# Which queue issues tile 1's keys and queries, and one zero product ahead of the first scores

## The reference

```python
scores = scale * np.matmul(q, k.transpose(0, 1, 3, 2))
keep = is_global | is_local          # 8 global keys, 96 local ones
scores = np.where(keep, scores + bias, -1e9)
a = exp(scores - max); a = a / (sum(a) + 1e-9); x = np.matmul(a, v)
h = x @ w_in; solu = h * softmax(h)
x = layer_norm(solu) * g_ln @ w_out
h = x @ w_in2; return (h * sigmoid(h)) @ w_out2
```

## Time and profile before

| | us |
|---|---|
| median of 3 runs | 492.46 (492.1 to 492.82) |
| the profiled execution | 491.45 |
| its span, first to last instruction | 489.4 |
| TensorE busy | 481.3 |
| VectorE, ScalarE, GpSimd busy | 303.5, 267.2, 228.9 |

### The profile page before, as it was taken

The page is one execution under the profiler, slowest core; times in us unless marked ns, Lnnn a source line. Parts: engine busy times, 40 slices in busy tenths (PEclk is TensorE's granted clock), DMA queues, the critical chain, the costliest instruction groups (busy, mean ns, idle before and its releaser), DMA issues.

```text
span 489.4 us, 8015 instructions
## 1 busy us (share of the span) xinstructions
PE 481.3 (98%) x2757; PEld 413.4 (84%) x2757; DVE 303.5 (62%) x729; ACT 267.2 (55%) x591; POOL 228.9 (47%) x304
## 2 busy tenths in 40 slices
PE   8989999999999999999999999999999999999997
PEld 6667888888888878888899988988899998988995
DVE  6877755675666777666575658565565546545542
ACT  5888556475566565745854454454454454344422
POOL 6626308779779779431624431444125431444100
PEclk9999999999999999999999999999999999999999
DMA  7994012642641641402222202221016202220003
GB/s 208 253 266 122 18 33 71 159 114 49 160 129 41 154 124 38 126 0 88 86 87 87 87 4 83 86 87 49 39 65 238 86 4 83 87 86 1 1 1 129
DMA packets 20522, 44.38 MB, mean 91 GB/s; under 512 B 2624, under 2 KB 8704, under 8 KB 20480
## 3 DMA queue, kind: packets, MB, share of 16 engines
q1 hardware_dynamic: 20160, 43.47, 30.7%
q10 hardware_dynamic: 320, 0.37, 0.3%
HBM read 40.69 MB, written 3.15 MB: 90 GB/s over the span
## 4 chain that ended last, share of the span: by engine, by line
PE 68%; POOL 18%; issue 4%; DVE 4%; SPq 3%; DMA 2%; ACT 1%; POOLq 0%
PE hidden_ps L1192 24%; PE score_ps L1215 9%; POOL k_split L703 7%; PE x_ps L1027 6%; POOL probs L730 5%; PE x_t_ps L1215 5%; PE x_ps L1215 5%; PE probs_t_ps L1215 5%; PE turn_ps L1215 5%; PE hidden_ps L978 3%; POOL k_split L701 3%; DVE solu L1763 2%; POOL q_lo L717 2%; DMA staged_q_raw<-q_t 2%; PE x_t_ps L965 2%
## 5 line engine op out<-in xcount | busy, mean ns | idle before, releaser
L873 POOL TENSOR_TENSOR wo_lo<-w_raw,wo_hi 128x512 fp32r<-128x512 f32 x32 | 41.4, 1312 | 145.6 <-ACT wo_hi L1461 145.6
L1473 ACT ACTIVATE act_hi<-mix_c 128x384 fp32r<-128x384 f32 x64 | 33.7, 526 | 96.5 <-DVE mix_c L1852 96.2
L730 POOL TENSOR_SCALAR probs<-probs,exp_inv 128x232 f32<-128x232 f32 x88 | 40.2, 474 | 43.6 <-DVE exp_inv L1623 41.6
L1295 ACT ACTIVATE probs<-logits,low_logit 128x232 f32<-128x232 f32 x96 | 45.5, 477 | 3.2 <-DVE low_logit L1610 2.9
L1852 DVE TENSOR_TENSOR mix_u<-hidden_ps,mix_p 128x384 f32<-128x384 f32 x16 | 8.9, 558 | 57.0 <-PE hidden_ps L1192 57.0
L1027 PE MATMUL x_ps<-w_out_hi,u_hi 128*128 128x512 f32 x96 | 40.5, 422 | 0.0
L1857 DVE TENSOR_TENSOR act_lo<-mix_c,act_hi 128x384 fp32r<-128x384 f32 x64 | 36.1, 567 | 6.3 <-ACT mix_c L1474 5.5
L1027 PE MATMUL x_ps<-w_out_hi,u_lo 128*128 128x512 f32 x96 | 37.9, 395 | 0.0
L1027 PE MATMUL x_ps<-w_out_lo,u_hi 128*128 128x512 f32 x96 | 37.6, 391 | 0.0
L978 PE MATMUL hidden_ps<-w_in_hi,x_hi 128*128 128x512 f32 x80 | 33.0, 412 | 0.0
L1474 ACT ACTIVATE mix_c<-mix_c 128x384 f32<-128x384 f32 x64 | 32.5, 508 | 0.0
(11 more groups left out here) (215 smaller groups left out, 1456.8 us busy)
## 6 DMA issues: line engine op xcount, KB each, us to landing
w_raw<-w SPq DMA_DIRECT2D x16, 1024.0 KB, 5.0
v_sb<-v_win SPq DMA_DIRECT2D x22, 224.0 KB
late_k_raw<-k_t SPq DMA_DIRECT2D x16, 232.0 KB, 4.4
k_raw<-k_t SPq DMA_DIRECT2D x14, 232.0 KB, 3.8
out<-out_sb SPq DMA_DIRECT2D x12, 256.0 KB, 2.1
w_in_raw<-w_in SPq DMA_DIRECT2D x4, 512.0 KB, 8.3
w_out_raw<-w_out SPq DMA_DIRECT2D x4, 512.0 KB, 12.4
late_q_raw<-q_t SPq DMA_DIRECT2D x16, 128.0 KB, 4.1
```

The costliest lines, as they stand in the source:

```text
L730: last = nc.gpsimd.tensor_scalar(probs[p][:, e, :], probs[p][:, e, :], exp_inv[:, p, e:e + 1], 0.0, ALU.mult, ALU.add)
L873: nc.gpsimd.tensor_tensor(wo_lo[j % 2][:, c, :], w2_raw[j % 2][:, c, BANK:2 * BANK], wo_hi[j % 2][:, c, :].bitcast(F32), ALU.subtract).the ...
L1295: last = nc.scalar.activation(probs[p][:, e, :], logits[b][:, e, :], ACT.Exp, scale=-1.0, bias=low_logit[:, b, e:e + 1], accum_out=exp_sum ...
L1473: nc.scalar.activation(act_hi[c][:, :], mix_c[c][:, :], ACT.Silu)
```

## The change

The function `load_early` moves out of SP's block so that any engine can run it, and takes the engine as an argument. The call for tile 1 is taken out of SP's list and put into ScalarE's, behind `load_first(act, 0)` and ahead of `first_table(0)`; the calls for tiles 2, 3 and 4 stay with SP. The first `keep_warm` has six products of zeros instead of seven.

```diff
--- before.py
+++ after.py
@@ -551,21 +551,20 @@
             eng.dma_start(staged_k_raw[rows, keys], k_v[0, unit][:, keys]).then_inc(loaded, 16)
             eng.dma_start(staged_q_raw[rows, queries], q_v[0, unit][:, queries]).then_inc(loaded, 16)
 
+    def load_early(eng, t):
+
+        if t in (2, 3):
+            eng.wait_ge(scores_done, PAIRS * (t - 1))
+        keys, queries = raw_of(t, 0)
+        for unit in range(2):
+            eng.dma_start(keys[unit * DH:unit * DH + DH, :], k_v[t, unit]).then_inc(early_loaded[t], 16)
+        for unit in range(2):
+            eng.dma_start(queries[unit * DH:unit * DH + DH, :], q_v[t, unit]).then_inc(early_loaded[t], 16)
+
     with nc.Block() as block:
 
         @block.sync
         def _(sp):
-            def load_early(t):
-
-
-                if t in (2, 3):
-                    sp.wait_ge(scores_done, PAIRS * (t - 1))
-                keys, queries = raw_of(t, 0)
-                for unit in range(2):
-                    sp.dma_start(keys[unit * DH:unit * DH + DH, :], k_v[t, unit]).then_inc(early_loaded[t], 16)
-                for unit in range(2):
-                    sp.dma_start(queries[unit * DH:unit * DH + DH, :], q_v[t, unit]).then_inc(early_loaded[t], 16)
-
             def load_keys_queries(t, s):
 
                 if not there(t):
@@ -615,7 +614,6 @@
 
             sp.dma_start(spans_i[:, :], spans).then_inc(spans_loaded, 16)
             load_first(sp, 1)
-            load_early(1)
             load_values(0, 0)
             load_values(0, 1)
             load_weight(0)
@@ -631,15 +629,15 @@
                 sp.dma_start(wide_q[:, :], wide_q_v[0, 0, 0]).then_inc(wide_stored, 16)
                 wide_heads(sp, wide_head)
             load_wide_x(0)
-            load_early(2)
+            load_early(sp, 2)
             load_weight(4)
             load_weight(5)
-            load_early(3)
+            load_early(sp, 3)
             load_values(2, 0)
             load_values(2, 1)
             load_weight(6)
             load_weight(7)
-            load_early(4)
+            load_early(sp, 4)
             load_keys_queries(WHOLE, 0)
             load_wide_x(1)
             load_wide_x(2)
@@ -1150,7 +1148,7 @@
             for _ in range(5):
                 nc.tensor.matmul(turn_ps[:, 0:P], x_hi[:, 0:P], x_hi[:, 0:P], start=True, stop=True)
             pe.wait_ge(zeros_made, 1)
-            keep_warm(7)
+            keep_warm(6)
             early_scores(0, 0)
             early_scores(0, 1)
             pe.wait_ge(identity_made, 1)
@@ -1484,6 +1482,7 @@
                                      bias=wide_stat[:, 0:1], accum_out=wide_stat[:, 1:2]).then_inc(wide_exp_done, 1)
 
             load_first(act, 0)
+            load_early(act, 1)
             first_table(0)
             first_table(1)
             exps(0, 0)
```

## The result

The changed kernel takes 494.58 us (median of 6 runs, 493.7 to 495.52) against 492.01 of the kernel before (6 runs, 491.48 to 492.82). The ratio is 1.0047, with a 95% interval of 1.0031 to 1.0062: slower, and outside the range given. The profiled execution took 494.52, its span is 492.5, which is 3.1 more than before. The medians lie only 2.6 apart: the profiled execution of the kernel before (491.45) was quicker than its median, so differences between the two sets of rows can come out some 0.5 us too large.

The account below looks back on a forecast made before the run. Loads bound the stage: tile 2's scores start at the later of A (25.46 - 0.30 = 25.16) and B (24.85), so 0.30 us earlier, taking the 492.46 median to 492.2 us. The 8-in-10 range was 491.4 to 493.2.

Parts of the forecast that it names:

- A: Time when tile 2 has landed and its scores can start: 25.46 before, forecast 25.16.
- B: Time when TensorE has finished the work ahead of tile 2's scores: 24.55 before, forecast 24.85.
- 0.91 of cover: TensorE's wait for tile 2's load, 24.55 to 25.46, claimed to hide delays in earlier work.
- no drain behind the table load: ScalarE's next activation follows the table load at once; the skill page's drain would make the kernel 0.8 us slower.
- the late first mask: VectorE's first mask at about 7.72 instead of 7.42, waiting for ScalarE's late bias tables: +0.30 us on following work.
- the product's place: One zero product fewer on TensorE: tile 0's first scores 0.46 us earlier, at 4.88, a gain not used later.
- the landing of tile 1: Tile 1's keys and queries, through ScalarE's queue, land at 9.5 instead of 10.4; harmless up to 10.7.
- Rival 3: ScalarE's queue gets only half the engines; tile 1 landing from 11.3 on costs time, at 12.2 493.35 us; chance 0.12.
- the favourable bound: Best case for tile 1's loads: data alone takes 3.0 us, so 8.0 plus a tail of 0.3 to 1.1.
- the second half of tile 0: Load for tile 0's later scores, taken as landed at 6.15, before the first half's passes end.
- rival 4: TensorE idle from 9.0 to 12.2 gets the lower clock again: up to 3 us, 495.5; chance 0.05.
- two stretches in which the engines were not full: DMA holes at 5.50 to 6.00 and 10.25 to 11.25, worth 0.20 and 0.23 us; filling them gains 0.30.

Follow-up runs that it names:

- SP held back: Changed kernel, but SP waits for tile 0's landing before issuing values and weights: 491.95 us, ratio 0.9992 to the kernel before; repeated, 491.74, ratio 0.9996.
- one-queue kernel: Kernel before with six zero products, SP issuing tile 1's loads behind tile 0's values instead of ahead: 493.4 us against 492.66, ratio 1.0018.
- split kernel: Changed kernel, but ScalarE issues unit 0 of tile 1 and SP unit 1 ahead of the values: 492.16 us against 492.66, ratio 0.9984.
- second experiment: Changed kernel with seven zero products put back, so only the loads move: 494.78 us, ratio 1.0045 to the kernel before.
- first experiment: Kernel before with six zero products instead of seven, tile 1's loads still on SP: 491.89 us against 492.16, ratio 0.9993.
- third experiment: Changed kernel with six more zero products between tile 0's score halves and twelve more before tile 1's scores: 493.63 us, ratio 1.0025 to the kernel before.
- the one that waits behind the values: Changed kernel, but SP issues tile 0's values, then waits for tile 0's landing before the first weight load: 493.93 us, ratio 1.0031 to the kernel before.

## Why the prediction was wrong

**Right.** That the stage is max(A, B) with 0.91 of cover in the profiled execution, and that TensorE runs almost through behind it. (Its waits of over 0.2 us do not all end by 32.50: the fifth, of 0.23 for GpSimd, ends at 172.03. It changes nothing.) The issue times (table load at 5.95 for 5.91; four issues of 0.62 with 0.04 between them are 2.60, as measured, and not 2.56), no drain behind the table load, the first scores at 4.92 for 4.88, the late first mask (7.88 for 7.72), and that the product's place brings nothing. With SP held back, ScalarE's late start costs what was worked out: TensorE was ready for tile 2 at 25.14 - 0.20 = 24.94 and at 26.09 - 1.10 = 24.99, for a B of 24.85.

**The step that failed** is the landing of tile 1. I took 9.5 "as the values ahead of it in SP's queue are only 0.48 MB", with 12.2 as the worst. It was 13.1. The 9.5 does not even follow from that premise: 0.74 and 0.48 MB at the 247 GB/s of the sum are 4.9 us, so 9.9 and, with the tail of 0.3 to 1.1, 10.2 to 11.0. The one-queue kernel, with just these values ahead, had tile 1 at 12.4. The larger error is in what shares the engines: not the loads ahead in the other queue, but all that this queue holds until the last byte lands, the weights behind the values included. The fair comparison was 0.75 MB of ScalarE's and 1.06 MB of SP's, over the 8 us that they took together. That the weights share in the delay follows from this count (1.06 MB is more than the 0.48 MB of values); no run held back the weights alone until tile 1 had landed. Rival 3 had the mechanism and its threshold (11.3), with a chance of 0.12 and a landing still 0.9 too early. By its own rule 13.1 gives B = 24.85 + 2.4 = 27.25, and +1.8; what the landing adds in the profiled execution, 2.67 less the 0.91 of cover, is about the same 1.8. Its chance was too low because I read the 28% for ScalarE's queue from 4.50 to 5.25 as a queue that had little left, and let the favourable bound stand nearer.

**A second miss** lies under it: the second half of tile 0 was taken as landed at 6.15, as before. It landed at 8.2. I had asked what shares the engines with the moved loads, and not what the moved loads share them with. Its wait of 1.46 us has no price of its own in these rows, as tile 1 came later still, but it is nearly all of the 1.69 us of idle time ahead of the clock's fall.

**The clock** was rival 4, tied to an idle stretch from 9.0 to 12.2 and given 0.05. It fell at 9.9, ahead of the wait for tile 1: behind the wait of 1.46 for tile 0's second half, the scores of that half and 0.23 more. It stayed low to 16.7, with the 1.93 of waiting for tile 1 inside. The split kernel had the same kind of wait for tile 0 (1.53), none for tile 1, and its clock was back by 13.0. Of the 4.0 us by which TensorE is behind at 16.98, 2.67 are there when tile 1's scores start, and 1.34 come in the stretch at the lower clock (scores 1.92 for 1.05, and the turn and zero products behind them). Less the cover of 0.91 that is 3.1, close to the growth of the span. The fall doesn't happen in every execution to the same degree: mean clocks were 0.992 to 0.997 in the changed kernel's runs, which lie 1.8 apart, and 0.989 to 0.999 in those of the second experiment, 3.8 apart. The two rivals were also not apart: late landings, tile 0's first of all, bring the idle time, and so their chances should have been one chance with both prices.

**Tile 2's landing (A)** was forecast 0.30 earlier, from two stretches in which the engines were not full. It came later instead:

```profile
L562 SPq DMA_DIRECT2D staged_q_raw<-q_t x1: 597/597/597, 13.0 to 13.0; - x1
...
DMA to landing us min/median/max: 13.7/13.7/13.7
```

Tile 2 landed at 13.0 + 13.7 = 26.7 in the profiled execution, 1.3 later than before. There it no longer mattered, as TensorE came at 28.47. But it means that even with B as forecast this execution would have started tile 2's scores 1.2 us late and not 0.30 early. Part of that may be the difference between executions, as the other kernels have 25.14 to 26.09 for a start that waits on this load. The first stretch did not fill: the DMA share from 2.00 to 6.50 is 0.71, where it was 0.85. Why more issued loads left the engines emptier is open; from 4.75 to 6.25 the one-queue kernel has 0.70 against 0.88 of the kernel before, so it is not the second queue as such.

## What to carry to other kernels

A second queue is no second set of engines. Before a load is moved to it, add up all that the first queue will hold from the issue of the moved load to its landing, and give each queue a share of the engines: a load on which an engine waits belongs where nothing unneeded is served beside it. Here a wait of the other queue on the urgent data, one line, brought back the whole loss. And where an engine's clock depends on its work, a wait that becomes longer can cost twice: once as the wait, and once in the slower work behind it. Count the waits of the loads that share engines with the moved ones too.

## What the runs showed of the hardware

The lower clock came although TensorE had been busy for half of the stretch before it (1.71 of 3.40 us). In the first experiment it was busy for 1.89 of the same 3.40 us (6.50 to 9.90), and the clock stayed at 1.00. The times spread more where the clock fell: 492.9 to 496.66 in the second experiment, with mean clocks of 0.989 to 0.999, against 493.1 to 494.2 where zero products filled the waits. That the clock is the whole reason is not shown: the second experiment's run at 0.999 took 495.54, and the kernel before lay between 490.74 and 494.36 in one session, with clocks of 0.995 to 1.0. The Trainium skill (TensorE: Matmul & The Clock Gate, section "Part 1: The HAM clock gate (the "warmup" mystery)") says that the throttled state is the default, which activity releases, and that the moment differs from run to run for the same kernel. The traces agree. Two kernels with the same work on TensorE up to the end of these passes, the third experiment and the one that waits behind the values, have these rows for the first eight passes of tile 0's scores:

```profile
4.92 1.05 PE L916 MATMUL score_ps<-staged_k_raw,staged_q_raw 64*128 64x232 f32 x8
```

```profile
4.91 1.92 PE L917 MATMUL score_ps<-staged_k_raw,staged_q_raw 64*128 64x232 f32 x8
```

In the one the clock had risen before them, in the other it had not when they were done. Neither kernel's edits lie ahead of these passes on TensorE. The profile's clock column does not tell them apart: it has 1.00 for both at that time.

The table load took 1.28 us in every trace, and the next activation started with its end (5.95, then 7.25). The Trainium skill (ScalarE: Activation LUTs, section "What ACT_TABLE_LOAD costs") has 2.66 us, the same load and a drain of about 1.38; the traces show the load and no drain.
